# An expert layer whose token rows are turned on VectorE instead of TensorE

## The chip, the cores and the metric

One core of one Trainium2 chip runs the whole program. The metric is the device time of one execution in microseconds (us). Engines are TensorE (matmuls; PE in the profile, its weight loads PEld), VectorE (DVE), ScalarE (ACT), GpSimd (POOL) and SyncE (SP), which issues most DMAs.

## The reference

Three stages in a row on 1536 tokens of 384 features, all fp32: a linear attention, a dense feed-forward layer, and a mixture of eight experts. The change touches the third stage (and the rows that enter it):

```python
def _moe2_ref(x, w_gate, w1, w2, capacity):      # x 1536x384, w1 8x384x1024, w2 8x1024x384
    logits = x @ w_gate
    expert_idx = np.argmax(logits, axis=1)
    ...
    # each expert takes its tokens in order of arrival, up to capacity (384)
    h = np.maximum(np.einsum('ecd,edf->ecf', disp, w1), 0.0)
    y = np.einsum('ecf,efd->ecd', h, w2)
    out[i] = gate_w[i] * y[expert_idx[i], pos[i]]
```

## The kernel before

Each engine has a program of its own, written out by hand, and semaphores tie them together. An engine executes its program in order: what stands behind a wait waits too.

The dense layer ends at about 264 us of the trace. GpSimd has by then scattered each token's row (384 features, its gate, its number) into `slots` in DRAM, by expert. From there the experts 0 to 7 are computed one after the other, 256 slots each (more tokens than that take a branch at the end, which this input doesn't use). Expert e = 2i + r uses the buffers of parity r: the weights of odd experts lie where the dense layer's weights were (`wd_*`), those of even ones in `we_*`. Expert 0 is computed in two tiles of 128 slots by code of its own (`tile_fc1`, `tile_fc2`, `pick_rows`); experts 1 to 7 by `expert(i, r, more)`, where `more` says that another one follows.

Every fp32 product is made of three fp32r matmuls: high by high, high by low, low by high. So each operand is split: ScalarE copies the high part (`_hi`), and VectorE or GpSimd subtracts to get the low part (`_lo`).

Inside an expert, f counts the eight tiles of 128 hidden features:

- TensorE: fc1(f), 9 matmuls of 256 columns into bank f % 2, then from f = 2 on fc2(f - 2), two tiles of slots t, 3 matmuls of 384 columns each, into `ps_ye[t]`. Behind f = F_X = 5 the six transposes `expert_x` of the next expert's rows `xrow` into `ps_xt`. Behind f = 7 come fc2(6) and fc2(7). fc1(f) waits for ge_lo(f - 2), whose bank it overwrites.
- ScalarE: ge_hi(f), the relu of fc1's bank. At f = 2, 3, 4 also a chunk each (1024 columns) of the next expert's W1, at f = 2 after a wait for W1's landing (`s_w1`). At f = 5 the copies of the next x, and from f = 5 on the chunks of W2 (wait `s_w2`).
- VectorE: ge_lo(f); behind it at f = 3, 4, 5 the low part of W1's chunk (L1308), at f = 5 also x_lo (L1293) and the copy of the tokens' numbers to `tok_i` (semaphore tok_ready). After f = 7 `yrow`, the result times the gate (L1321, semaphore ye_ready).
- GpSimd: the low parts of W2's three chunks, then the scatter of the two tiles of `yrow` to `out`.
- SyncE: for each expert the loads of the expert two further on into the buffers of the same parity: W1 (1.5 MB) when all its fc1 are done (he_done), W2 (1.5 MB) when its last fc2 is done (fc2e_done), and the rows x when yrow and tokens have been taken:

```python
                    sp.wait_ge(s_he, ET * (2 * i + r + 1))
                    load_w(2 * i + 2 + r, r)
                    sp.wait_ge(s_fc2e, ET * (2 * i + r + 1))
                    load_w2(2 * i + 2 + r, r)
                    sp.wait_ge(s_ye[r], 2 * (i + 1))
                    sp.wait_ge(s_tok[r], i + 1)
                    load_x(2 * i + 2 + r, r)
```

Of the kernel before, what the change touches and what calls it, by code (L numbers as in the profile page):

```python
# [7 lines left out]
ALU = mybir.AluOpType  # L8
# [4 lines left out]
def build(nc, B, H, S, D, DFF, NE, FE, CAP, rkt_in, nat_in, decay, bonus, bonus_pair, win, wout, wouttr, wgate, wexp, out, slots):  # L13
# [5 lines left out]
    DM = H * D  # L19
# [37 lines left out]
    NOVER = NE + 3  # L57
    LATE = NE * CAP
# [39 lines left out]
    x2t = new("x2t", [128, BT, DM])  # L98
    lg = new("lg", [128, BT, NE])
# [32 lines left out]
    def expert_rows(r):  # L132
        return (new(f"xrow{r}", [128, 2, XR]), new(f"xe_hi{r}", [128, KT, SN], F32R),
                new(f"xe_lo{r}", [128, KT, SN], F32R), new(f"yrow{r}", [128, 2, DM]),
                new(f"tok_i{r}", [128, 2, 1], U32))
# [8 lines left out]
    xrow, xe_hi, xe_lo, yrow, tok_i = zip(rows0, expert_rows(1))  # L144
# [32 lines left out]
    with ctx:  # L177
# [268 lines left out]
        def _(sp):  # L446
# [330 lines left out]
        def _(act):  # L777
# [204 lines left out]
        def _(dve):  # L982
# [273 lines left out]
            def tokens_of(t, s):  # L1256
                dve.wait_ge(s_xr[0], 16 * (t + 1))
                V.tensor_copy(tok_i[0][:, t, :], xrow[0][:, t, TOKEN:XR]).then_inc(s, 1)

            def gated(t, y):  # L1260
                V.tensor_scalar(yrow[0][:, t, :], y, xrow[0][:, t, GATE:GATE + 1], None, ALU.mult).then_inc(s_ye[0], 1)
# [25 lines left out]
            dve.wait_ge(s_y0, 1)  # L1287
            gated(0, ps_y[0][:, 0:DM])

            def expert_x(i, r):  # L1290
                for c, (src, dst) in enumerate(((ps_xt[0][:, :], (0, 2)), (ps_xt[1][:, 0:SN], (2, 3)))):
                    dve.wait_ge(s_xehi[r], 2 * i + c + 1)
                    V.tensor_tensor(xe_lo[r][:, dst[0]:dst[1], :], src.rearrange("p (k n) -> p k n", n=SN),  # L1293
                                    xe_hi[r][:, dst[0]:dst[1], :].bitcast(F32), ALU.subtract).then_inc(s_xelo[r], 1)

            def expert(i, r, more):
                ni, nr = (i, 1) if r == 0 else (i + 1, 0)
                for f in range(ET):
# [17 lines left out]
                for t in range(2):  # L1316
                    if t == 0:
                        dve.wait_ge(s_y0, 2 * i + r + 1)
                    else:
                        dve.wait_ge(s_fc2e, ET * (2 * i + r + 1))  # L1320
                    V.tensor_scalar(yrow[r][:, t, :], ps_ye[t][:, 0:DM], xrow[r][:, t, GATE:GATE + 1], None,  # L1321
                                    ALU.mult).then_inc(s_ye[r], 1)

            tile_row(s_he, ET, s_lrow)
# [10 lines left out]
            dve.wait_ge(s_fc2e, ET)  # L1335
            gated(1, ps_y[0][:, 0:DM])
            expert(0, 1, True)
            with dve.Fori(1, NE // 2 - 1) as i:
                expert(i, 0, True)
                expert(i, 1, True)  # L1340
            expert(NE // 2 - 1, 0, True)
            expert(NE // 2 - 1, 1, False)
# [21 lines left out]
        def _(pe):  # L1364
# [292 lines left out]
            def pick_rows():  # L1657

                pe.wait_ge(s_xr[0], 32)
                for kt in range(KT):  # L1660
                    mm(ps_s[0][:, 128 * kt:128 * kt + 128], xrow[0][:, 1, 128 * kt:128 * kt + 128], ident[:, :],
                       start=kt == 0, stop=False, skip_group_check=True)
                pe.wait_ge(s_pick, 1)
                rows = x2row[(NB - 1) % 2]
                for kt in range(KT):
                    for t in range(BT):
                        last = mm(ps_s[0][:, 128 * kt:128 * kt + 128], rows[:, t, NE + 128 * kt:NE + 128 * kt + 128],
                                  picked[:, t, :], start=False, stop=kt == KT - 1 and t == BT - 1,
                                  skip_group_check=True)
# [14 lines left out]
            def expert_x(i, r):  # L1684
                pe.wait_ge(s_xr[r], 32 * (i + 1))
                if r:
                    pe.wait_ge(s_xelo[0], 2 * (i + 1))
                else:
                    wait_if(pe, s_xelo[1], 2 * i)
                for kt in range(KT):  # L1690
                    for t in range(2):
                        at = (kt % 2) * SN + t * 128
                        last = nc.tensor.transpose(ps_xt[kt // 2][:, at:at + 128],  # L1693
                                                   xrow[r][:, t, 128 * kt:128 * kt + 128], ident[:, :])
                last.then_inc(s_xtr[r], 1)

            def fc2_expert(i, r, f, tiles=(0, 1)):
                pe.wait_ge(s_gelo, ET * (2 * i + r) + f + 1)
                if f == 0:
                    pe.wait_ge(s_ehi[r], 2 * N1 * (i + 1))  # L1700
                    wait_if(pe, s_elo2[r], N1 * (i + r))
                    y_before, n_before = other(s_ye, r, i)
                    wait_if(pe, y_before, 2 * n_before)
                cols = slice(W1 + f * DM, W1 + (f + 1) * DM)
                for t in tiles:
                    g = slice(t * 128, (t + 1) * 128)
# [7 lines left out]
            def expert(i, r, more):  # L1714
                ni, nr = (i, 1) if r == 0 else (i + 1, 0)

                pe.wait_ge(s_elo1[r], N1 * (i + 1) + (0 if r else N1))
                for f in range(ET):
                    q = ET * (2 * i + r) + f
                    wait_if(pe, s_gelo, q if f == 0 else q - 1)  # L1720
# [23 lines left out]
                    if more and f == F_X:  # L1744
                        expert_x(ni, nr)
                if more:
                    fc2_expert(i, r, ET - 2)
                    fc2_expert(i, r, ET - 1)
                else:
# [12 lines left out]
            expert_x(0, 1)  # L1762
# [7 lines left out]
            expert(0, 1, True)  # L1770
            with pe.Fori(1, NE // 2 - 1) as i:
                expert(i, 0, True)
                expert(i, 1, True)
            expert(NE // 2 - 1, 0, True)
            expert(NE // 2 - 1, 1, False)
            pe.wait_ge(s_over, 1)
            over = pe.value_load(n_over[0:1, 0:1], min_val=0, max_val=T)
            with pe.If(over > SN):
                with pe.Fori(0, NOVER) as e:
                    pe.wait_ge(s_dld, 32 * (e + 1))  # L1780
                    for kt in range(KT):
                        last = nc.tensor.transpose(ps_xt[0][:, 128 * kt:128 * kt + 128],
                                                   xrow[0][:, 0, 128 * kt:128 * kt + 128], ident[:, :])
# [93 lines left out]
```

## Time and profile before

| | |
|---|---|
| median of three runs | 415.0 us (414.7 to 415.39) |
| the profiled execution | 415.56 us |
| its span in the trace | 413.7 us |
| TensorE busy | 406.2 us (98%) |
| VectorE, ScalarE, GpSimd busy | 242.4, 188.1, 231.4 us |
| granted TensorE clock | 0.997 of full speed |
| experts 1 to 6 | 285.85 to 391.91 us |

The span is the profiler's, from the first instruction to the last; the execution's own time is longer by what lies around it. Matmuls are pipelined: one of 256 columns is shown as 0.28 us long, but the next starts 0.12 behind it. So the start-to-start distance is what a matmul costs. The same holds to a lesser degree on VectorE and ScalarE, where the next instruction starts up to 0.1 before the end of the last. A wait shows as idle time in brackets with what ended it.

### The profile page before, as it was taken

The page shows a single profiled execution, that of the slowest core. Times are in us where ns is not written, and L with a number is a line of the kernel's source. Part 1 is how long each engine was busy: PE and PEld are TensorE (multiplying, and loading weights), DVE is VectorE, ACT ScalarE, POOL GpSimd, SP SyncE. Part 2 cuts the span into 40 slices and gives each one's busy share as a digit, 9 for nine tenths or more (in the row PEclk, how much of TensorE's full clock was granted, in tenths as well). Part 3 has the DMA queues.
Part 4 walks back from the last instruction along what each step waited for, and adds up shares of the span by engine and source line. Part 5 has one row for each costly group of instructions (what it writes and reads, how often), then busy time and mean ns, then how long its engine had stood idle before and what let it go on. Part 6 is the DMA issues. An engine that isn't in the chain of part 4 may idle for free.

```text
span 413.7 us, 9445 instructions
## 1 busy us (share of the span) xinstructions
PE 406.2 (98%) x3697; PEld 390.3 (94%) x3697; DVE 242.4 (59%) x576; ACT 188.1 (45%) x409; POOL 231.4 (56%) x239
## 2 busy tenths in 40 slices
PE   8999999999999999999999999999999999999995
PEld 8799799999999999999999999999999999999995
DVE  7787955376576547654663487785635546364522
ACT  4786553233333333333343455552645455474420
POOL 3789865567856685668234336065083562826531
PEclk9999999999999999999999999999999999999998
DMA  7998997214030403020018001827383845729000
GB/s 281 399 395 341 348 371 255 72 49 150 10 119 2 139 21 118 2 87 21 2 19 345 2 2 38 326 77 238 135 304 99 346 147 217 279 100 363 8 31 28
DMA packets 18650, 64.98 MB, mean 157 GB/s; under 512 B 2203, under 2 KB 11717, under 8 KB 16432
## 3 DMA queue, kind: packets, MB, share of 16 engines
q1 hardware_dynamic: 16672, 59.67, 39.5%
q0 software_dynamic: 1792, 4.73, 3.0%
q8 instruction: 28, 0.46, 0.5%
q14 instruction: 14, 0.11, 0.1%
q10 hardware_dynamic: 144, 0.00, 0.0%
HBM read 51.98 MB, written 13.21 MB: 158 GB/s over the span
## 4 chain that ended last, share of the span: by engine, by line
PE 88%; DVE 4%; issue 3%; DMA 3%; POOL 1%; ACT 1%; POOLq 0%; SPq 0%; DVEq 0%
PE bank L1369 26%; PE bank L1371 25%; PE bank L1370 24%; PE bank L1390 2%; DMA xrow<-slots 2%; PE bank L1419 1%; PE bank L1455 1%; PE bank L1459 1%; PE bank L1693 1%; PE bank L1448 1%; PE bank L1451 1%; PE bank L1546 1%; PE bank L1728 1%; PE bank L1729 1%; PE bank L1632 1%
## 5 line engine op out<-in xcount | busy, mean ns | idle before, releaser
L707 POOL TENSOR_TENSOR g_lo<-elu,g_hi 128x256 fp32r<-128x256 f32 x95 | 73.7, 777 | 86.9 <-ACT g_hi L882 86.6
L1369 PE MATMUL bank<-xt,wd_hi 128*128 128x256 f32 x285 | 80.5, 283 | 0.6 <-DVE elu L1197 0.6
L1371 PE MATMUL bank<-xt,wd_lo 128*128 128x256 f32 x285 | 80.4, 282 | 0.0
L1370 PE MATMUL bank<-xt,wd_hi 128*128 128x256 f32 x285 | 80.3, 282 | 0.0
L873 ACT ACTIVATE elu<-elu 128x256 f32<-128x256 f32 x96 | 40.1, 418 | 76.4 <-DVE elu L1189 75.9
L1369 PE MATMUL bank<-wd_hi,g_hi 128*128 128x392 f32 (+1 forms) x192 | 67.4, 351 | 0.0
L1371 PE MATMUL bank<-wd_hi,g_lo 128*128 128x392 f32 (+1 forms) x192 | 65.2, 340 | 0.0
L1370 PE MATMUL bank<-wd_lo,g_hi 128*128 128x392 f32 (+1 forms) x192 | 65.1, 339 | 0.0
L1197 DVE SCALAR_TENSOR_TENSOR elu<-elu,bank 128x256 f32<-128x256 f32 x96 | 40.3, 419 | 41.1 <-ACT elu L873 41.1
L882 ACT CAST g_hi<-elu 128x256 fp32r<-128x256 f32 x96 | 39.0, 406 | 44.1 <-DVE elu L1197 44.1
L1369 PEld LDWEIGHTS bank<-xt,wd_hi 128*128 128x128 f32 x285 | 53.9, 189 | 1.2 <-DVE elu L1197 1.1
L1371 PEld LDWEIGHTS bank<-xt,wd_lo 128*128 128x128 f32 x285 | 54.1, 190 | 0.0
L1370 PEld LDWEIGHTS bank<-xt,wd_hi 128*128 128x128 f32 x285 | 54.0, 189 | 0.0
L1301 DVE SCALAR_TENSOR_TENSOR ge_lo<-bank,ge_hi 128x256 fp32r<-128x256 f32 x56 | 23.8, 424 | 48.8 <-ACT ge_hi L940 48.8
L1189 DVE TENSOR_SCALAR elu<-bank 128x256 f32<-128x256 f32 x80 | 33.8, 422 | 31.2 <-PE bank L1371 26.3
L940 ACT ACTIVATE ge_hi<-bank 128x256 fp32r<-128x256 f32 x56 | 21.6, 385 | 53.4 <-PE bank L1371 31.5
L724 POOL TENSOR_TENSOR wd_lo<-wd_raw,wd_hi 128x1024 fp32r<-128x1024 f32 x12 | 30.4, 2559 | 27.5 <-ACT wd_hi L953 24.5
L1369 PEld LDWEIGHTS bank<-wd_hi,g_hi 128*128 128x128 f32 x192 | 36.3, 189 | 2.0 <-POOL g_lo L707 0.8
L724 POOL TENSOR_TENSOR we_lo<-we_raw,we_hi 128x1024 fp32r<-128x1024 f32 x9 | 21.3, 2402 | 27.6 <-ACT we_hi L953 27.6
L1370 PEld LDWEIGHTS bank<-wd_lo,g_hi 128*128 128x128 f32 x192 | 36.4, 190 | 0.0
L1371 PEld LDWEIGHTS bank<-wd_hi,g_lo 128*128 128x128 f32 x192 | 36.0, 188 | 0.0
L729 POOL DMA_INDIRECT out<-yrow,tok_i x16 | 15.7, 982 | 17.4 <-DVE yrow L1321 11.7
(220 smaller groups left out, 943.7 us busy)
## 6 DMA issues: line engine op xcount, KB each, us to landing
we_raw<-wexp SPq DMA_DIRECT2D x8, 1536.0 KB, 6.5
wd_raw<-wexp SPq DMA_DIRECT2D x8, 1536.0 KB, 7.4
rkt<-rkt SPq DMA_DIRECT2D x12, 512.0 KB, 5.7
nat<-nat SPq DMA_DIRECT2D x9, 672.0 KB, 5.4
xrow<-slots SPq DMA_DIRECT2D x16, 193.0 KB, 7.4
wd_raw<-win SPq DMA_DIRECT2D x4, 768.0 KB, 8.6
wd_raw<-wout SPq DMA_DIRECT2D x4, 768.0 KB, 9.0
wo_tr<-wouttr SPq DMA_DIRECT2D x1, 3072.0 KB, 17.6
```

The source lines that it names most:

```text
L707: nc.gpsimd.tensor_tensor(g_lo[:, f % 4, :], elu[:, f % 2, :], g_hi[:, f % 4, :].bitcast(F32), ALU.subtract).then_inc(s_glo, 1)
L724: nc.gpsimd.tensor_tensor(EL[r][:, cols], ER[r][:, cols], EH[r][:, cols].bitcast(F32), ALU.subtract).then_inc(s_elo2[r], 1)
L729: nc.gpsimd.indirect_dma_start(out=out, out_offset=bass.IndirectOffsetOnAxis(ap=tok_i[r][:, t, :], axis=0), in_=yrow[r][:, t, :], in_offse ...
L873: nc.scalar.activation(elu[:, f % 2, :], elu[:, f % 2, :], ACT.Exp, scale=-1.0 if n == 0 else 1.0).then_inc(s_exp, 1)
L882: nc.scalar.copy(g_hi[:, f % 4, :], elu[:, f % 2, :]).then_inc(s_ghi, 1)
L940: nc.scalar.activation(ge_hi[:, f % 4, :], ps_e[f % 2][:, 0:SN], ACT.Relu).then_inc(s_gehi, 1)
L1189: V.tensor_scalar_min(elu[:, f % 2, :], ps_h[f % 2][:, 0:BN], 0.0).then_inc(s_m, 1)
L1197: V.scalar_tensor_tensor(out=elu[:, f % 2, :], in0=elu[:, f % 2, :], scalar=-1.0, in1=ps_h[f % 2][:, 0:BN], op0=ALU.add, op1=ALU.max).then ...
L1301: V.scalar_tensor_tensor(out=ge_lo[:, f % 4, :], in0=ps_e[f % 2][:, 0:SN], scalar=0.0, in1=ge_hi[:, f % 4, :].bitcast(F32), op0=ALU.max, o ...
L1369: mm(dst, w_hi, x_hi, start=start, stop=False)
L1370: mm(dst, w_hi, x_lo, start=False, stop=False)
L1371: return mm(dst, w_lo, x_hi, start=False, stop=stop)
```

## The change

**The rows' load.** `load_x` brought 256 rows in two DMAs of 128 rows. Now the rows come in blocks: four DMAs, each of which brings columns 96p to 96p + 95 of all 256 rows to the 32 partitions from 32p on, row 32b + i to partition 32p + i, block b; and a fifth for gate and token number. In SyncE's loop the load of x stands first, and it waits for the token copy alone.

**The transpose.** TensorE's `expert_x` is gone. VectorE's `expert_cols` turns all 24 squares of 32 by 32 with one instruction, from `xrow` to `xcol` (the storage of `x2t`, free by then), at f = 4. To make 96 columns fill 32 partitions, feature 3q + k becomes row q of the k-th third; the weights W1 are put in the same order by the host (`thirds`), and expert 0's matmul transposes read every third column (`block_cols`).

**The gates.** A copy of the gates to `gate`, beside that of the tokens, so that `xrow` is free earlier.

**The seam.** fc2(6) and fc2(7) of an expert come behind fc1(0) and fc1(1) of the next; VectorE's yrow (`expert_out`) moves behind ge_lo(1) of the next. The first fc2 waits for W2's chunks one by one and for each `ps_ye[t]` by itself.

```diff
+        def block_cols(rows, kt):
+            return rows.rearrange("p (m k) -> p k m", k=KT)[:, kt, :]
+        def xrow_blocks(r):
+            return xrow[r][:, :, :].rearrange("p t c -> p (t c)")[:, 0:2 * DM].rearrange("p (b c) -> p b c", b=8)
...
             def load_x(e, r):
-                for t in range(2):
-                    sp.dma_start(xrow[r][:, t, :],
-                                 slots[bass.ds(e * CAP + t * 128, 128), :]).then_inc(s_xr[r], 16)
+                for p in range(4):
+                    sp.dma_start(xrow_blocks(r)[32 * p:32 * p + 32, :, :],
+                                 slots[bass.ds(e * CAP, SN), 96 * p:96 * p + 96]
+                                 .rearrange("(b i) c -> i b c", i=32)).then_inc(s_xr[r], 16)
+                sp.dma_start(xrow_gt(r), slots[bass.ds(e * CAP, SN), GATE:XR]
+                             .rearrange("(t p) c -> p t c", t=2)).then_inc(s_xr[r], 16)
...
                 for r in range(2):
+                    sp.wait_ge(s_tok[r], i + 1)
+                    load_x(2 * i + 2 + r, r)
                     sp.wait_ge(s_he, ET * (2 * i + r + 1))
                     load_w(2 * i + 2 + r, r)
                     sp.wait_ge(s_fc2e, ET * (2 * i + r + 1))
                     load_w2(2 * i + 2 + r, r)
-                    sp.wait_ge(s_ye[r], 2 * (i + 1))
-                    sp.wait_ge(s_tok[r], i + 1)
-                    load_x(2 * i + 2 + r, r)
...
+            def expert_cols(i, r):
+                dve.wait_ge(s_xr[r], rows_loaded(i, r))
+                V.transpose(xcol.rearrange("p k (b n) -> p b k n", n=32),
+                            xrow_blocks(r).rearrange("p b (n k) -> p b k n", k=KT)).then_inc(s_xtr[r], 1)
...
+                    if f == 1 and behind:
+                        expert_out(bi, br)
...
+                    if more and f == F_X - 1:
+                        expert_cols(ni, nr)
                     if more and f == F_X:
                         expert_x(ni, nr)
                     if f == 5:
-                        dve.wait_ge(s_xr[r], 32 * (i + 1))
+                        dve.wait_ge(s_xr[r], rows_loaded(i, r))
                         wait_if(dve, s_sout[r], 32 * i)
-                        V.tensor_copy(tok_i[r][:, :, :], xrow[r][:, :, TOKEN:XR]).then_inc(s_tok[r], 1)
+                        V.tensor_copy(gate[r][:, :, :], xrow_gt(r)[:, :, 0:1])
+                        V.tensor_copy(tok_i[r][:, :, :], xrow_gt(r)[:, :, 1:2]).then_inc(s_tok[r], 1)
...
+            expert_cols(0, 1)
             tile_row(s_he, ET, s_lrow)
...
                     last.then_inc(s_he, 1)
+                    if f < 2 and behind:
+                        fc2_expert(bi, br, ET - 2 + f)
                     if more and f >= 2:
                         fc2_expert(i, r, f - 2)
...
-                    if more and f == F_X:
-                        expert_x(ni, nr)
-                if more:
-                    fc2_expert(i, r, ET - 2)
-                    fc2_expert(i, r, ET - 1)
```

SyncE's queue, one turn of its loop for the even experts, before (an ISA row computes an address and holds the waits; `wexp` are the weights in DRAM, columns 0 to 3071 W1, the rest W2):

```order
L516 ISA [waits he_done]
L516 DMA we_raw<-wexp 128x3072
L519 ISA [waits fc2e_done]
L519 DMA we_raw<-wexp 128x3072
L552 ISA
L523 ISA [waits tok_ready0,ye_ready0]
L523 DMA xrow_90<-slots 128x386
L523 ISA
L523 DMA xrow_90<-slots 128x386
```

and now:

```order
L537 ISA [waits tok_ready0]
L537 DMA xrow_90<-slots 32x8x96
...
L537 DMA xrow_90<-slots 32x8x96
L540 ISA
L540 DMA xrow_90<-slots 128x2x2
L567 ISA
L530 ISA [waits he_done]
L530 DMA we_raw<-wexp 128x3072
L533 ISA [waits fc2e_done]
L533 DMA we_raw<-wexp 128x3072
```

Five x DMAs and the wait for tok_ready now stand ahead of the wait for he_done and of W1's DMA; they stood behind W2's.

VectorE's queue in the loop, from ge_lo(4) of an even expert to the token copy, before:

```order
L1301 SCALAR_TENSOR_TENSOR ge_lo<-bank,ge_hi 128x256 [waits ge_hi_ready]
L1306 REGISTER_ALU
L1308 TENSOR_TENSOR wd_lo<-wd_raw,wd_hi 128x1024 [waits we_hi_ready1]
L1292 REGISTER_ALU
L1293 TENSOR_TENSOR xe_lo_100<-bank,xe_hi_99 128x512 [waits xe_hi_ready1]
...
L405 REGISTER_ALU [waits xrow_loaded0]
L1315 CAST tok_i_94<-xrow_90 128x2 [waits out_scattered0]
```

and now (the pair of ge_lo and split shown first is that of f = 4):

```order
L1334 SCALAR_TENSOR_TENSOR ge_lo<-bank,ge_hi 128x256 [waits ge_hi_ready]
L1341 REGISTER_ALU
L1343 TENSOR_TENSOR wd_lo<-wd_raw,wd_hi 128x1024 [waits we_hi_ready1]
L1309 ISA
L1310 STREAM_TRANSPOSE x2t<-xrow_99 128x8x3x32 [waits xrow_loaded1]
L1333 REGISTER_ALU
L1334 SCALAR_TENSOR_TENSOR ge_lo<-bank,ge_hi 128x256 [waits ge_hi_ready]
...
L1316 TENSOR_TENSOR xe_lo_101<-x2t,xe_hi_100 128x512 [waits xe_hi_ready1]
...
L1352 COPY gate_95<-xrow_90 128x2 [waits out_scattered0]
L1353 CAST tok_i_94<-xrow_90 128x2
```

The transpose stands ahead of ge_lo(5), the gate copy ahead of the token copy, and x_lo reads the scratchpad instead of a bank.

## Rows read from the trace of the kernel before

**Rows 1.** The page, busy us of each engine, share, instructions.

```profile
PE 406.2 (98%) x3697; PEld 390.3 (94%) x3697; DVE 242.4 (59%) x576; ACT 188.1 (45%) x409; POOL 231.4 (56%) x239
```

**Rows 2.** Timeline of TensorE: start, us, line, operation, out<-in.

```profile
285.85 0.28 PE L1728 MATMUL bank<-xe_hi,wd_hi 128*128 128x256 f32 x1
...
391.91 0.28 PE L1728 MATMUL bank<-xe_hi,wd_hi 128*128 128x256 f32 x1
```

**Rows 3.** Chain that ended last: start, us, what.

```profile
296.67 0.66 PE bank L1693 x6
```

**Rows 4.** TensorE's timeline at a seam, and the chain inside fc2.

```profile
287.83 0.28 PE L1371 MATMUL bank<-xe_hi,wd_lo 128*128 128x256 f32 x1
288.00 0.38 PE L1369 MATMUL bank<-xe_hi,wd_hi 128*128 128x256 f32 x1
...
372.06 0.17 PE bank L1369
```

**Rows 5.** Timeline of TensorE, second tile of expert 0.

```profile
279.95 0.82 PE L1693 MATMUL bank<-ident,xrow 128*128 128x128 f32 x6
280.90 0.66 PE L1632 MATMUL bank<-ident,hrow 128*128 128x128 f32 x4
```

**Rows 6.** Issue to landing, W1 (L516), then W2 (L519), six each.

```profile
DMA to landing us min/median/max: 6.1/6.4/7.7
...
DMA to landing us min/median/max: 6.7/7.9/9.0
```

**Rows 7.** Who waited for whom, 285 to 414: us, times, longest.

```profile
ACT wd_hi L945 <- DMA wd_raw<-wexp: 1.0, 1, 1.0
```

**Rows 8.** Timeline of ScalarE, 298 to 299.

```profile
298.10 1.06 ACT L953 CAST we_hi<-we_raw 128x1024 fp32r<-128x1024 f32 x1
299.06 0.39 ACT L940 ACTIVATE ge_hi<-bank 128x256 fp32r<-128x256 f32 x1
```

**Rows 9.** Timeline of VectorE, 280 to 304, idle before in brackets.

```profile
280.15 0.69 DVE L1249 TENSOR_SCALAR hrow<-bank 128x512 f32<-128x512 f32 x1 [1.23 <-PE bank L1371]
...
283.87 0.14 DVE L1258 CAST tok_i<-xrow 128x1 uint32<-128x1 f32 x1
...
293.97 0.42 DVE L1301 SCALAR_TENSOR_TENSOR ge_lo<-bank,ge_hi 128x256 fp32r<-128x256 f32 x1 [0.54 <-ACT ge_hi L940]
294.31 1.22 DVE L1308 TENSOR_TENSOR we_lo<-we_raw,we_hi 128x1024 fp32r<-128x1024 f32 x1
...
297.98 1.02 DVE L1293 TENSOR_TENSOR xe_lo<-bank,xe_hi 128x512 fp32r<-128x512 f32 x2 [0.35 <-ACT xe_hi L932]
298.91 0.16 DVE L1315 CAST tok_i<-xrow 128x2 uint32<-128x2 f32 x1
...
303.12 1.14 DVE L1321 TENSOR_SCALAR yrow<-bank,xrow 128x384 f32<-128x384 f32 x2 [1.77 <-PE bank L1371]
```

**Rows 10.** VectorE by line: count, busy us, mean ns; splits of W1.

```profile
L1285 DVE TENSOR_TENSOR wd_lo<-wd_raw,wd_hi 128x1024 fp32r<-128x1024 f32 x3 | 5.7, 1955 | 0.0
...
L1308 DVE TENSOR_TENSOR wd_lo<-wd_raw,wd_hi 128x1024 fp32r<-128x1024 f32 x9 | 10.9, 1215 | 0.0
```

**Rows 11.** Timeline of SyncE, 280 to 305, DMA issues.

```profile
280.33 0.35 SPq L516 DMA_DIRECT2D we_raw<-wexp  x1
...
300.65 0.33 SPq L516 DMA_DIRECT2D wd_raw<-wexp  x1
...
304.44 0.86 SPq L523 DMA_DIRECT2D xrow<-slots  x2
```

**Rows 12.** DMA packets between 1.9 and 2.4 us, the startup.

```profile
DMA packets 282, 0.03 MB, mean 69 GB/s; under 512 B 275, under 2 KB 275, under 8 KB 282
```

**Rows 13.** Timeline of GpSimd, the scatter of expert 1's first tile.

```profile
306.52 0.99 POOL L729 DMA_INDIRECT out<-yrow,tok_i  x1 [0.16 <-issue]
```

**Rows 14.** Expert 1's x DMAs: ns, starts, landing.

```profile
L523 SPq DMA_DIRECT2D xrow<-slots x2: 327/381/435, 272.9 to 273.3; - x2
...
DMA to landing us min/median/max: 2.6/2.6/2.7
```

More of the change, by code:

```diff
@@ L143, in build @@
     ge_lo = new("ge_lo", [128, 4, SN], F32R)
-    xrow, xe_hi, xe_lo, yrow, tok_i = zip(rows0, expert_rows(1))
+    xrow, xe_hi, xe_lo, yrow, tok_i, gate = zip(rows0, expert_rows(1))
     wo_tr, end_g = put("wo_tr", [128, KT, DFF], F32, wo_at)
@@ L1287, in _, with expert_out, expert @@
             dve.wait_ge(s_y0, 1)
+            dve.wait_ge(s_atok, 1)
             gated(0, ps_y[0][:, 0:DM])
+            def expert_cols(i, r):
+                dve.wait_ge(s_xr[r], rows_loaded(i, r))
+                V.transpose(xcol.rearrange("p k (b n) -> p b k n", n=32),
+                            xrow_blocks(r).rearrange("p b (n k) -> p b k n", k=KT)).then_inc(s_xtr[r], 1)
             def expert_x(i, r):
-                for c, (src, dst) in enumerate(((ps_xt[0][:, :], (0, 2)), (ps_xt[1][:, 0:SN], (2, 3)))):
+                for c, (lo, hi) in enumerate(((0, 2), (2, 3))):
                     dve.wait_ge(s_xehi[r], 2 * i + c + 1)
-                    V.tensor_tensor(xe_lo[r][:, dst[0]:dst[1], :], src.rearrange("p (k n) -> p k n", n=SN),
-                                    xe_hi[r][:, dst[0]:dst[1], :].bitcast(F32), ALU.subtract).then_inc(s_xelo[r], 1)
-            def expert(i, r, more):
+                    V.tensor_tensor(xe_lo[r][:, lo:hi, :], xcol[:, lo:hi, :],
+                                    xe_hi[r][:, lo:hi, :].bitcast(F32), ALU.subtract).then_inc(s_xelo[r], 1)
+            def expert_out(i, r):
+                dve.wait_ge(s_tok[r], i + 1)
+                for t in range(2):
+                    if t == 0:
+                        dve.wait_ge(s_y0, 2 * i + r + 1)
+                    else:
+                        dve.wait_ge(s_fc2e, ET * (2 * i + r + 1))
+                    V.tensor_scalar(yrow[r][:, t, :], ps_ye[t][:, 0:DM], gate[r][:, t, :], None, ALU.mult).then_inc(s_ye[r], 1)
+            def expert(i, r, more, behind):
                 ni, nr = (i, 1) if r == 0 else (i + 1, 0)
+                bi, br = (i - 1, 1) if r == 0 else (i, 0)
                 for f in range(ET):
@@ L1312, in expert @@
                     if f == 5:
-                        dve.wait_ge(s_xr[r], 32 * (i + 1))
+                        dve.wait_ge(s_xr[r], rows_loaded(i, r))
                         wait_if(dve, s_sout[r], 32 * i)
-                        V.tensor_copy(tok_i[r][:, :, :], xrow[r][:, :, TOKEN:XR]).then_inc(s_tok[r], 1)
[L1316 to L1322, printed above, removed]
+                        V.tensor_copy(gate[r][:, :, :], xrow_gt(r)[:, :, 0:1])
+                        V.tensor_copy(tok_i[r][:, :, :], xrow_gt(r)[:, :, 1:2]).then_inc(s_tok[r], 1)
+                if not more:
+                    expert_out(i, r)
+            expert_cols(0, 1)
             tile_row(s_he, ET, s_lrow)
@@ L1682, in _, with w2_chunk @@
             last.then_inc(s_y0, 1)
[L1684 to L1695, printed above, removed]
+            def w2_chunk(f):
+                return -(-(f + 1) * DM // ECH)
             def fc2_expert(i, r, f, tiles=(0, 1)):
                 pe.wait_ge(s_gelo, ET * (2 * i + r) + f + 1)
[L1699 to L1703, printed above, removed]
+                if w2_chunk(f) > w2_chunk(f - 1):
+                    pe.wait_ge(s_ehi[r], 2 * N1 * (i + 1) - N1 + w2_chunk(f))
+                    wait_if(pe, s_elo2[r], N1 * (i + r) - N1 + w2_chunk(f))
                 cols = slice(W1 + f * DM, W1 + (f + 1) * DM)
                 for t in tiles:
+                    if f == 0:
+                        y_before, n_before = other(s_ye, r, i)
+                        pe.wait_ge(y_before, 2 * n_before - 1 + t)
                     g = slice(t * 128, (t + 1) * 128)
@@ L1712, in fc2_expert, with expert @@
                     last.then_inc(s_fc2e, 1)
-            def expert(i, r, more):
+            def expert(i, r, more, behind):
                 ni, nr = (i, 1) if r == 0 else (i + 1, 0)
+                bi, br = (i - 1, 1) if r == 0 else (i, 0)
                 pe.wait_ge(s_elo1[r], N1 * (i + 1) + (0 if r else N1))
@@ L1743, in expert @@
                                 fc2_expert(i, r, f - 2 - t, (t,))
-                    if more and f == F_X:
-                        expert_x(ni, nr)
-                if more:
-                    fc2_expert(i, r, ET - 2)
-                    fc2_expert(i, r, ET - 1)
-                else:
+                if not more:
                     for t in range(2):
@@ L1850 @@
     w_in = moe_w_in[order].reshape(DM // 128, 128, DFF // 128, 128).transpose(1, 2, 0, 3).reshape(128, -1)
+    thirds = [DM // 128 * p + kt for kt in range(DM // 128) for p in range(128)]
     gate_pad = np.zeros((DM, 32), np.float32)
```

49 lines of the change are left out of this document (28 added, 21 removed).

## Prediction

> **What bounds the kernel now.** I read the page first: TensorE is busy 98% of the span and no other engine above 59% [rows 1], so the kernel is a row of matmuls and every other engine matters only through what it makes TensorE wait for. Then TensorE's timeline over the seven experts: the first fc1 matmul of expert 1 starts at 285.85 and that of expert 7 at 391.91 [rows 2]. That is 106.06 us for six periods, 17.68 each. The chain of waits shows what the change can take out of a period: six transposes of expert rows, 0.66 [rows 3]. At the seam next to nothing is lost: from the last matmul of fc1(1) to the first of fc1(2) is 0.17 in all, of which I count 0.05 as idle [rows 4]. So if all else kept up, six periods would lose 6 x 0.71 = 4.3 us. The first transposes, at 279.95, win nothing: they lie inside TensorE's wait for hrow, which lasts to 280.90 either way [rows 5].
>
> **The part that moves.** The stream of weights has next to no slack. ScalarE waits for W1 of the next expert at f=2, in line ahead of ge_hi(3). Before, W1 is issued 0.3 behind the last fc1 and lands 6.1 to 7.7 later, median 6.4 [rows 6]; once already ScalarE sat 1.0 on it [rows 7]. Now SyncE's queue holds, ahead of that W1, a wait for tok_ready of the current expert and five DMAs. tok_ready comes from VectorE at f=5, behind everything that hangs on the W1 just landed: the split of the chunks, the transpose, x_lo, two copies. So a ring closes: W1 lands, ScalarE, VectorE, token copy, SyncE, five x DMAs, next W1. Its length, not TensorE's, is the period when it is longer than TensorE's 17.0 (17.68 less 0.71).
>
> **The ring's length, step by step.** From W1's landing: ScalarE splits chunk 0, and ge_hi(3) starts 0.96 behind it (298.10 to 299.06) and takes 0.38 [rows 8]; with 0.05 to wake and 0.04 to VectorE, ge_lo(3) starts at +1.43. VectorE then never rests. ge_lo to the next instruction is 0.34 (293.97 to 294.31); a split is 1.22 busy [rows 9, 10] and, with the same 0.08 of overlap, 1.14 start to start; x_lo is 0.93 (297.98 to 298.91) [rows 9]. Three ge_lo 1.02, three splits 3.42, x_lo 0.93, gate copy and token copy 0.25.
>
> The transpose has no row. 768 columns at a split's rate (1024 in 1215 ns) [rows 10] are 0.91 in proportion, an estimated 0.95 busy with a fixed part, 0.87 start to start: the low end, since an instruction that reads and writes each column once has nothing to gain on the split. The high end is 1.8, twice that, if 4-byte data in strided blocks go at half rate; the splits that ran beside GpSimd, 1955 ns instead of 1215 [rows 10], are the only row of such a slowing. I take 0.87, as the row with most alike (fp32, scratchpad to scratchpad, one stream out). Sum from landing to token copy: 1.43 + 1.02 + 3.42 + 0.93 + 0.25 + 0.87 = 7.9. Then 0.2 to the first x DMA, as from yrow's end at 304.26 to 304.44 [rows 9, 11].
>
> X, the delay of W1 by the five x DMAs. Two of the old ones stand 0.53 apart (0.86 for both, each 0.33) [rows 11], so five cost 2.65 in issue alone: the low end. They hold 1280 pieces (4 x 256 of 384 B, 256 of 8 B) where the old two held 256. In the startup 282 packets of two queues, 275 of them under 512 B, came in 0.5 us [rows 12]: 1.8 ns a packet, or about 3.6 for one queue. At that rate 1280 pieces keep the queue 4.6 us, and W1 stands behind them: the high end. I take 3.4, nearer to the issue pace, since a startup of two queues at once is a poor row for a rate.
>
> W, issue to landing of W1: 6.1 to 7.7 [rows 6]. I take 6.8, above the median, because W1, issued 3 to 4 later than before, now flies while GpSimd scatters two tiles of out; before they began at 306.52, 5.9 behind W1's issue at 300.65 [rows 13, 11]. W2's landings, which share the queue with such traffic, range from 6.7 to 9.0 [rows 6].
>
> The Trainium skill (DMA: Bandwidth & Descriptors, Specifications) wants at least 512 B for line rate and says that below this a read-modify-write is done; its section on the anatomy of one DMA calls descriptor generation small, with many descriptors before the cost shows. By the second alone X would be the 2.65 of issue and the sum +0.1, no change; by the first X moves to its high end. No row here shows a load of this kind.
>
> **The sum.** Write Z = X + W = 10.2. The first token copy of the ring, for expert 0, ends at 283.87 + 0.14 [rows 9], 284.35 with the gate copy (0.15) and the wake (0.2). This one is worse than later ones: W1 of expert 2 was issued right behind the last fc1 of expert 0, at 280.33 [rows 11]. Now it lands at 284.35 + 10.2 = 294.55. Each later W1 lands 8.1 + 10.2 = 18.3 behind the one ahead; the sixth, for expert 7, at 386.05. Expert 7 starts when ge_lo(6) of expert 6 is done, which stands right behind the token copy: 7.9 + 0.4 later, 394.35. At that point 12 fc2 matmuls are still owed that before lay ahead of the seam, 12 x 0.17 = 2.1 [rows 4]. So 394.35 + 2.1 - 391.91 = +4.5. In general it is 6Z - 56.7: no change at Z = 9.4; TensorE's own pace, and no further gain, from about Z = 8.7; with a slower transpose add 6 x the excess. The tail behind expert 7's start has no transposes and keeps its length.
>
> **Costed at nothing.** The deferred fc2(6) and fc2(7) are as many matmuls as before. expert_out moves behind ge_lo(1); its two yrow, 1.14 together [rows 9], fit before fc2(0) wants the banks, by about 0.3, since TensorE has 2.1 of work in between; if late, each lateness is TensorE's. The x loads themselves land long before f=4 of the next expert. The softer waits on W2's chunks win nothing where no W2 wait is seen, and W2, behind W1 in the queue, is wanted only after x_hi. The early transposes of expert 0's rows now read their stationary side every third column: 21 matmuls of 0.11 (six take 0.66) [rows 3], doubled, are +2.3 at the worst; at equal cost 0. I take 0, since the loads of the weights overlap the matmuls. expert_cols(0, 1) stands ahead of hrow on VectorE, which was free 1.23 there, up to hrow's start at 280.15 [rows 9]; the x rows, issued from 272.9 and landing in 2.6 [rows 14], now X later, are there at 278.9, and the transpose ends at 279.85, 0.3 before hrow's start; at the high end of X it is a microsecond late.
>
> **Time.** The profiled execution took 415.56 for a span of 413.7; the median of the runs is 415.0, and I add to that: **419.5 us**.
>
> **Rivals.** (a) *Faster.* Z stays under 9.4: five issues cost 2.65 and W1 lands in 6.1 to 6.6. Then Z = 8.75 to 9.25, the change -4.3 to -1.2: 410.7 to 413.8. For it: the median of 6.4 and the issue pace [rows 6, 11]. Against: it needs pieces of 384 B to cost nothing and no scatter in W1's way. 0.26. (b) *No change*, Z within 0.15 of 9.4: 0.06. (c) *The forecast*, Z from 9.6 to 11.5, 416 to 427: 0.54. (d) *Worse*: the transpose at 1.8 gives +5.6 more, 425; both X and W at their high ends, 4.6 + 7.7 = 12.3, give +17, 432. 0.14. The low and high ends together are 410.7 and 432, and 437 with the slow transpose. (e) That the transposes don't leave TensorE can't be: the order shows them gone.
>
> A gain or loss under 0.2% (0.8 us) is what a measurement can't tell from no change. **Range** 411 to 428: about 1 in 10 lies under it, inside (a), and 1 in 10 above, inside (d). The forecast case alone is 416 to 427. Slower 0.68, same 0.06, faster 0.26.
>
> **What would show it.** Right: ScalarE waits of 3 to 5 us for W1 by DMA at L945 and its twin in each expert but the last; W1 issued 3 or more behind the last fc1; TensorE idle about 1 in each period, at fc1(5) or at the next expert's start on ge_lo, and first fc1s 18.3 apart. Each term is a row: transpose 0.95, five issues, W1's landing. Wrong: first fc1s 17.0 apart and no ScalarE wait (a), or a transpose row near 1.8 (d). What would make it wrong otherwise is a stall of hrow over 1 us, or expert_out blocking fc2(0).

## The result, and the profile after

The changed kernel takes 431.19 us (median of 5 runs, 430.24 to 431.94) against 415.22 (5 runs beside it): 1.0384 times the time before [1.0373, 1.0396]. The forecast was 419.5, range 411 to 428. The direction came true, the size did not: the loss is 16.0 us, not 4.5. Of the six executions of the experiment w_x_w2_gate_f4 below, two (425.62, which is the profiled one, and 428.04) lie over 1.5% above its fastest and are left out of its time and ratio.

The page of the changed kernel, against [rows 1]: TensorE is as busy as before in microseconds and idle for the rest; VectorE is 18 us busier, far more than seven transposes and seven copies should cost.

```profile
PE 407.0 (95%) x3655; PEld 389.6 (91%) x3655; DVE 260.7 (61%) x592; ACT 187.0 (44%) x409; POOL 232.9 (54%) x239
```

TensorE's timeline after, first fc1 matmul of experts 1, 2, 4 and 7 (before: [rows 2]):

```profile
286.80 0.28 PE L1755 MATMUL bank<-xe_hi,wd_hi 128*128 128x256 f32 x1
...
306.69 0.57 PE L1755 MATMUL bank<-xe_hi,we_hi 128*128 128x256 f32 x1 [2.25 <-DVE ge_lo L1334]
...
345.73 0.38 PE L1755 MATMUL bank<-xe_hi,we_hi 128*128 128x256 f32 x1 [2.26 <-DVE ge_lo L1334]
...
404.66 0.35 PE L1755 MATMUL bank<-xe_hi,wd_hi 128*128 128x256 f32 x1 [1.55 <-issue]
```

The six periods are 117.86 in all, 11.80 more than the 106.06 before. The 2.07 of fc2 work that the new order puts behind each seam is still owed at that point, and expert 1 starts 0.95 later: 11.80 + 2.07 + 0.95 = 14.8, which is the growth of the span (413.7 to 428.5).

The waits of the changed kernel, 270 to 430 us (engine, line, releaser: us in all, times, longest), against [rows 7]: ScalarE now waits for W1 for each of the six experts, as predicted, for 1.5 to 5.3.

```profile
ACT we_hi L961 <- DMA we_raw<-wexp: 11.0, 3, 5.3
...
ACT wd_hi L961 <- DMA wd_raw<-wexp: 6.4, 3, 2.8
PE bank L1755 <- DVE ge_lo L1334: 7.7, 4, 2.3
```

One turn of the ring can be read off four timelines. ScalarE, the start and the end of the turn (W1 has just landed in both):

```profile
335.07 1.05 ACT L961 CAST we_hi<-we_raw 128x1024 fp32r<-128x1024 f32 x1 [2.89 <-DMA we_raw<-wexp]
...
354.50 1.05 ACT L961 CAST wd_hi<-wd_raw 128x1024 fp32r<-128x1024 f32 x1 [2.84 <-DMA wd_raw<-wexp]
```

VectorE between them:

```profile
336.43 0.42 DVE L1334 SCALAR_TENSOR_TENSOR ge_lo<-bank,ge_hi 128x256 fp32r<-128x256 f32 x1 [3.80 <-ACT ge_hi L956]
...
339.37 1.21 DVE L1310 STREAM_TRANSPOSE x2t<-xrow 128x768 f32<-128x768 f32 x1
340.50 0.38 DVE L1334 SCALAR_TENSOR_TENSOR ge_lo<-bank,ge_hi 128x256 fp32r<-128x256 f32 x1
340.80 1.21 DVE L1343 TENSOR_TENSOR we_lo<-we_raw,we_hi 128x1024 fp32r<-128x1024 f32 x1
341.93 1.02 DVE L1316 TENSOR_TENSOR xe_lo<-x2t,xe_hi 128x512 fp32r<-128x512 f32 x2
342.87 2.33 DVE L1352 COPY gate<-xrow 128x2 f32<-128x2 f32 x1
345.12 0.16 DVE L1353 CAST tok_i<-xrow 128x2 uint32<-128x2 f32 x1
```

GpSimd (the first of its three splits of W2) and SyncE at the same place:

```profile
342.58 2.59 POOL L740 TENSOR_TENSOR we_lo<-we_raw,we_hi 128x1024 fp32r<-128x1024 f32 x1 [8.45 <-ACT we_hi L969]
```

```profile
345.47 1.84 SPq L537 DMA_DIRECT2D xrow<-slots  x4
347.49 0.40 SPq L540 DMA_DIRECT2D xrow<-slots  x1
348.14 0.35 SPq L530 DMA_DIRECT2D wd_raw<-wexp  x1
```

The turn is 10.40 from the landing to the first x DMA, 2.67 to W1's issue and 6.36 to the landing: 19.43, where 8.1, 3.4 and 6.8 were predicted. The row that nobody expected is the gate copy: two columns, 2.33 us. It starts 0.29 behind GpSimd's first split of W2 and ends at 345.20, 0.03 behind the end of that split at 345.17. In six of seven experts it is so; in the last, beside which no split runs, it takes 0.16 (count, then ns least/median/most):

```profile
L1352 DVE COPY gate<-xrow x7: 158/2331/2360, 303.8 to 416.7; 128x2 f32<-128x2 f32 x7
```

### The profile page after: what moved, and what is told of

It reads as the page before. It is cut to its first block, busy times and chain, and to the rows that moved or that the text cites. A ratio compares the mean times of both kernels' runs of the same rounds, so it can differ in the third digit from the quotient of the medians.

```text
span 428.5 us, 9450 instructions
## 1 busy us (share of the span) xinstructions
PE 407.0 (95%) x3655; PEld 389.6 (91%) x3655; DVE 260.7 (61%) x592; ACT 187.0 (44%) x409; POOL 232.9 (54%) x239
## 4 chain that ended last, share of the span: by engine, by line
PE 74%; DVE 11%; issue 6%; DMA 5%; ACT 1%; SPq 1%; POOL 1%; DVEq 0%; POOLq 0%; ACTq 0%
PE bank L1404 21%; PE bank L1406 20%; PE bank L1405 20%; DMA we_raw<-wexp 3%; PE bank L1425 2%; DMA wd_raw<-wexp 2%; DVE we_lo L1343 1%; DVE gate L1352 1%; PE bank L1454 1%; DVE wd_lo L1343 1%; DVE xe_lo L1316 1%; PE bank L1490 1%; PE bank L1494 1%; DVE ge_lo L1334 1%; DVE x2t L1310 1%
## 5 line engine op out<-in xcount | busy, mean ns | idle before, releaser
L1334 DVE SCALAR_TENSOR_TENSOR ge_lo<-bank,ge_hi 128x256 fp32r<-128x256 f32 x56 | 22.8, 415 | 58.8 <-ACT ge_hi L956 58.8
```

## The experiments

Time and ratio of each are against the kernel before, run on the same chip.

**gate_f4** moves the gate copy from f = 5 to f = 4, right behind the transpose.

```diff
+                    if f == F_X - 1:
+                        dve.wait_ge(s_xr[r], rows_loaded(i, r))
+                        V.tensor_copy(gate[r][:, :, :], xrow_gt(r)[:, :, 0:1])
                     if more and f == F_X:
...
-                        V.tensor_copy(gate[r][:, :, :], xrow_gt(r)[:, :, 0:1])
```

> The changed kernel with one edit: the gate copy stands at f = 4 behind the transpose, before GpSimd begins its splits, instead of at f = 5. Theory A (a closed ring from W1's landing over the token copy to the next W1 sets the period, and the gate copy, held up 2.2 us while GpSimd splits W2, is a link of it): the copy takes 0.15, six periods of 19.4 to 19.9 shrink by 2.2 each to about 17.2, the time falls by 13, from 431.2 to about 418. Theory B (the ring is set by the five x DMAs and W1's landing, and the gate copy only fills time that would be waited anyway): the copy is short and the time stays within 1 us of 431.

Measured: 434.56 us, 1.0464 [1.0418, 1.051], slower still; both theories missed. The copy itself is 0.12 at its new place, but the block moved on to its neighbours. VectorE:

```profile
340.15 0.12 DVE L1349 COPY gate<-xrow 128x2 f32<-128x2 f32 x1
...
341.65 3.22 DVE L1316 TENSOR_TENSOR xe_lo<-x2t,xe_hi 128x512 fp32r<-128x512 f32 x2
344.80 2.30 DVE L1355 CAST tok_i<-xrow 128x2 uint32<-128x2 f32 x1
```

The token copy, now the first copy there, takes 2.30 to 2.36 in all six turns. In two of them, the one shown and the fifth, x_lo is blocked as well: its two pieces take 3.22 instead of 1.02, and the token copy behind it stands through the next split. From one landing of W1 to the next it is 19.5 to 19.9, and 21.6 and 22.0 in those two turns. So x_lo and a cast pay too; it isn't the gate copy's own doing.

**gate_cast** makes the gate tile fp32r, so that the copy is a cast; the two readers of the tile take it back as fp32. The gates are rounded by it.

```diff
-new(f"gate{r}", [128, 2, 1]))
+new(f"gate{r}", [128, 2, 1], F32R))
```

> The changed kernel with the gate copy left at f = 5 but written as fp32r (so the gates are rounded to that type): the instruction becomes a CAST like the token copy behind it, with the same source, size and place. If what is held up by GpSimd is this kind of instruction (a plain fp32 COPY from scratchpad to scratchpad), the row takes 0.15 and the time is about 418, as with the copy at f = 4. If any instruction of VectorE at that place waits for GpSimd's split (or for the source), it still takes 2.3 and the time stays at 431.

Measured: 432.09 us, 1.0392 [1.0366, 1.0419], as the changed kernel. The cast is blocked like the copy:

```profile
342.69 2.35 DVE L1352 CAST gate<-xrow 128x2 fp32r<-128x2 f32 x1
344.95 0.16 DVE L1353 CAST tok_i<-xrow 128x2 uint32<-128x2 f32 x1
```

**w_x_w2** opens the ring: SyncE issues W1 first, then waits for tok_ready.

```diff
-                    sp.wait_ge(s_tok[r], i + 1)
-                    load_x(2 * i + 2 + r, r)
                     sp.wait_ge(s_he, ET * (2 * i + r + 1))
                     load_w(2 * i + 2 + r, r)
+                    sp.wait_ge(s_tok[r], i + 1)
+                    load_x(2 * i + 2 + r, r)
```

> The changed kernel with one edit in SyncE's loop: wait he_done and W1's DMA first, then the wait for tok_ready and the five x DMAs, then W2; the gate copy stays at f = 5. Theory A: the ring is cut, W1 is issued 0.35 behind the last fc1 again and ScalarE waits under 0.5 for it. The gate copy, started about 1.3 before GpSimd's first chunk ends, then costs about 0.1 to 0.3 a period. Periods about 17.1, time 412 to 413. Theory B (small pieces slow the weights behind them in the queue, wherever they stand): W2 lands late instead, ScalarE waits for W2 at f = 5, time 416 or more.

Measured: 418.45 us, 1.0072 [1.0056, 1.0089]. ScalarE's waits for W1 are gone and with them 12.7 us, as theory A has it. Its time of 412 to 413 was missed: the gate copy is still 2.35, here at 354.14, and delays ge_lo(6), for which TensorE waits 0.9 to 1.0 in each of the six periods where 0.1 to 0.3 was expected. So the ring and the block are two things. Outside the ring the block makes a period 18.0 instead of the 16.8 of early (below), 1.2 more; inside it costs 2.3 (pool_waits). TensorE:

```profile
356.94 0.39 PE L1755 MATMUL bank<-xe_hi,wd_hi 128*128 128x256 f32 x1 [0.90 <-DVE ge_lo L1334]
```

**w_x_w2_gate_f4** is both edits.

> Both edits: SyncE issues W1, x, W2, and the gate copy stands at f = 4. Theory A: TensorE sets the period, 17.0 (17.68 less six transposes of 0.66 and the seam), so 6 x 0.7 = 4.2 under the kernel before, plus 1.0 which the strided weight loads of expert 0's rows cost: 411.5 to 412.3. Theory B: as without the gate edit, 416 or more.

Measured: 418.6 us in the median of four, 1.0083 [1.0066, 1.01]. Theory A was missed, as in gate_f4: in the one trace the token copy takes 2.30 to 2.36 in all six turns, and x_lo 3.25 in two. Theory B had the time but not the cause: no wait of ScalarE for a weight shows.

**pool_waits** leaves VectorE and SyncE as changed, and makes GpSimd wait with its W2 splits until the current expert's token copy is done.

```diff
             with pool.Fori(1, NE // 2 - 1) as i:
+                pool.wait_ge(s_tok[0], i + 1)
                 split_w2(i, 1)
                 scatter_out(i, 0)
+                pool.wait_ge(s_tok[1], i + 1)
                 split_w2(i + 1, 0)
```

(and likewise for the first and the last)

> The changed kernel with one edit, on GpSimd alone: it waits for tok_ready of the current expert before it begins the splits of W2. The two runs before moved the gate copy and changed its kind, and the 2.3 us moved to x_lo and to the token copy behind it. Theory A: a VectorE instruction that reads the scratchpad by both ports can't start while a split on GpSimd runs and waits for that one instruction's end (up to 2.4 us). With GpSimd held back, gate copy and token copy take 0.15 each and x_lo 1.0, each ring is 2.2 shorter, 17.2 instead of 19.4, and the time is 431.2 - 13 = about 418, though GpSimd starts later. Theory B: it is the read of xrow itself (a small strided piece that DMA wrote) or a short instruction behind x_lo that takes 2.3: the rows stay at 2.3 and the time at 431.

Measured: 417.40 us, 1.0051 [1.0035, 1.0066]: 13.8 us back from the changed kernel, 6 x 2.3. VectorE, then GpSimd right behind it:

```profile
373.52 0.16 DVE L1356 COPY gate<-xrow 128x2 f32<-128x2 f32 x1
373.58 0.16 DVE L1357 CAST tok_i<-xrow 128x2 uint32<-128x2 f32 x1
```

```profile
373.92 7.11 POOL L740 TENSOR_TENSOR we_lo<-we_raw,we_hi 128x1024 fp32r<-128x1024 f32 x3 [8.02 <-DVE tok_i L1357]
```

No instruction of VectorE, ScalarE or SyncE was changed; only GpSimd's splits start later, behind the token copy instead of 0.29 ahead of the gate copy. That shows the cause of the excess: a 128x2 copy of VectorE that starts behind one of GpSimd's splits isn't done until that split ends.

**early** keeps the change's SyncE order and moves VectorE's and ScalarE's x work ahead of GpSimd's splits: transpose at f = 2, gate copy, token copy and x_hi at f = 3, x_lo at f = 4. VectorE's part of the edit (ScalarE's `expert_x` moves from F_X to F_X - 2):

```diff
-                    if more and f == F_X - 1:
+                    if more and f == F_X - 3:
                         expert_cols(ni, nr)
-                    if more and f == F_X:
+                    if more and f == F_X - 1:
                         expert_x(ni, nr)
-                    if f == 5:
+                    if f == F_X - 2:
                         dve.wait_ge(s_xr[r], rows_loaded(i, r))
```

> The changed kernel with VectorE's and ScalarE's pieces drawn forward inside an expert, SyncE's order as in the change: transpose at f = 2, gate and token copies and x_hi at f = 3, x_lo at f = 4, all before GpSimd's splits begin. Theory A: no VectorE row is held up, tok_ready comes 3 us behind W1's landing, so the ring is 3.1 + 0.2 + 2.7 + 6.4 = 12.4 and binds nobody; TensorE sets the period at 17.0. Time 415.1 - 6 x 0.7 + 1.0 (strided weight loads for expert 0) = 411.5 to 412.3. Theory B (small pieces slow W1, or the transpose or the deferred work holds TensorE up somewhere else): ScalarE still waits for W1, 415 or more.

Measured: 415.56 us, 1.0002 [0.9993, 1.0011], no difference from before. First fc1s are 16.80 apart in five of the six periods (323.07, 339.87, ... 390.27), but 19.07 in the first: W1 of expert 2 still stands behind expert 0's token copy and five x DMAs, and ScalarE waits 5.4 for it. The expectation of 411.5 to 412.3 had left that one turn out; without the wait that period is 14.86 (early_w_first).

**early_natural** also reads expert 0's rows in contiguous columns, with a copy of expert 0's weights laid out for it (entry NE + 1 of `wexp`); the other experts are untouched.

```diff
-block_cols(xrow[0][:, 0, 0:DM], kt), ident[:, :])
+xrow[0][:, 0, 128 * kt:128 * kt + 128], ident[:, :])
...
-            load_w(0, 0)
+            load_w(NE + 1, 0)
```

> As the kernel with the pieces drawn forward, and expert 0 reads its rows in the natural order of features (contiguous stationary operand), with a copy of its weights in that order from the host. If the 0.95 us by which expert 1 starts later in the changed kernel (286.80 against 285.85) are the 21 transposes and picks with every third column as stationary operand, they go back to 0.11 each and the time is 0.9 to 1.1 under the kernel without this edit, 410.5 to 411.3. If the delay has another source (the transpose ahead of hrow), nothing changes.

Measured: 414.57 us, 0.9981 [0.9972, 0.999]: 1.0 less than early, as expected. TensorE grouped by line and shape, 262 to 290 us (count | busy us, mean ns), the changed kernel:

```profile
L1702 PE MATMUL bank<-picked,x2row 128*128 128x128 f32 x12 | 2.3, 338 | 0.0
...
L1696 PE MATMUL bank<-ident,xrow 128*128 128x128 f32 x6 | 1.2, 328 | 0.0
```

and early_natural:

```profile
L1702 PE MATMUL bank<-picked,x2row 128*128 128x128 f32 x12 | 1.5, 275 | 0.0
...
L1696 PE MATMUL bank<-ident,xrow 128*128 128x128 f32 x6 | 0.8, 274 | 0.0
```

**turn_plain** is early_natural with a transpose that reads 32 neighbouring columns. It leaves out the order by thirds: the features of experts 1 to 7 then stand in another order than the weights', so the output is another.

```diff
-rearrange("p b (n k) -> p b k n", k=KT)).then_inc(s_xtr[r], 1)
+rearrange("p b (k n) -> p b k n", k=KT)).then_inc(s_xtr[r], 1)
```

> As the one before, but VectorE's transpose reads 32 neighbouring columns per square instead of every third, so that the experts' features are in the wrong order. If the strided read is why 768 columns take 1.22 us (768 at a split's rate would be 0.95), the row falls to about 0.95. If the squares of 32 by 32 cost it, the row stays at 1.2.

Measured, one run: 414.49 us. The transposes of the two kernels, early_natural first (ns, least/median/most):

```profile
L1310 DVE STREAM_TRANSPOSE x2t<-xrow x7: 1216/1218/1247, 279.1 to 378.4; 128x768 f32<-128x768 f32 x7
```

```profile
L1310 DVE STREAM_TRANSPOSE x2t<-xrow x7: 962/967/969, 279.1 to 378.3; 128x768 f32<-128x768 f32 x7
```

Read contiguously it is about the 0.95 of the prediction; every third column costs 0.25 more. Off the ring, as here, that is worth nothing that one run shows (414.57 with the stride).

**early_w_first** is early_natural with SyncE's first turn taken out of the loop: for expert 2 alone W1 goes ahead of the token wait and the x DMAs (`True` in `loads`).

```diff
+            loads(0, 0, True)
+            loads(0, 1)
+            with sp.Fori(1, NE // 2 - 1) as i:
+                loads(i, 0)
+                loads(i, 1)
```

> The kernel with the pieces drawn forward and expert 0 in natural order, and SyncE's first turn taken out of the loop: for expert 2 it issues W1 ahead of the x rows, since expert 0's token copy comes late (285) and its last fc1 early (280). In the kernel without this edit ScalarE waits 5.2 us for that W1 and TensorE stands 2.4 + 1.2 in the first period, 18.82 instead of 16.8 + what is deferred. Theory A: those 3.6 us go, six periods of 16.8, expert 7 starts near 385.4: 414.6 - 3.6 = 411.0, 1.0% under the kernel before. Rival: the x rows of expert 2, now behind its W1 in the queue, land too late for the transpose at f = 2 of expert 1, and VectorE's wait gives back 1 us or more: 412 or above.

Measured: 410.44 us (409.88 to 410.66) beside 415.76, 0.987 [0.9853, 0.9886]: faster than both kernels, by 1.3% and 4.8%. SyncE's first turn, and the page:

```profile
280.38 0.35 SPq L530 DMA_DIRECT2D we_raw<-wexp  x1
284.35 1.90 SPq L537 DMA_DIRECT2D xrow<-slots  x4
```

```profile
PE 400.2 (98%) x3655; PEld 385.1 (94%) x3655; DVE 249.5 (61%) x592; ACT 188.5 (46%) x409; POOL 234.4 (57%) x239
```

TensorE is back at 98%, and the span is 4.1 less than early_natural's (408.7 and 412.8), where 3.6 was expected. The five full periods are 16.80 each. Before they were 17.68 in the mean, 17.6 to 17.7 but for the last, 17.93, in which ScalarE waits 1.0 for W1. So taking the transposes off TensorE and changing the seam, which no run here tells apart, is worth 0.8 to 0.9 a period once nothing else is late.

**x_in_ten** loads the same x rows in ten DMAs instead of five, in pieces of the same size and number.

```diff
-                for p in range(4):
+                for half in range(2):
+                    for p in range(4):
+                        b = slice(4 * half, 4 * half + 4)
```

> The changed kernel with the same x rows in ten DMAs instead of five (each half of the slots by itself), the same 1024 pieces of 384 B and 256 of 8 B. Theory A: what the x rows add to the ring is the time to issue them, 0.54 each, and not their pieces: W1 is issued 5.3 to 5.5 behind the token copy instead of 2.7, still lands 6.4 later, each ring is 2.7 longer, 22.1, and the time 431.2 + 6 x 2.7 = 447. Rival: the pieces set it (1280 at 3.6 ns), the issues lie inside that time, and the time stays within 3 us of 431.

Measured: 450.96 us, 1.0854 [1.0836, 1.0872], 19.8 more than the changed kernel. SyncE:

```profile
333.52 1.84 SPq L539 DMA_DIRECT2D xrow<-slots  x4
335.54 0.35 SPq L542 DMA_DIRECT2D xrow<-slots  x1
336.09 1.82 SPq L539 DMA_DIRECT2D xrow<-slots  x4
338.09 0.35 SPq L542 DMA_DIRECT2D xrow<-slots  x1
338.72 0.35 SPq L530 DMA_DIRECT2D we_raw<-wexp  x1
339.26 0.33 SPq L533 DMA_DIRECT2D we_raw<-wexp  x1
```

From the first x DMA to W1's issue it is 5.20, 2.53 more, and 6 x 2.53 = 15.2 (expected 6 x 2.7). The ring passes on each DMA issued in it; the count of issues is X, not the pieces. The other 4.6 go with W1's landing, which was expected to stay: ScalarE starts on it 7.5 behind its issue in the mean of six, against 6.8 in the changed kernel (6 x 0.8 = 4.7). The traces show what goes with it. In five of these turns W2's DMA is issued 0.5 behind W1's, as shown, and in four of the five W1 takes 7.8 to 8.5 (6.8 in the other). In the changed kernel that is so in the first turn alone, with 8.1; where W2 comes 2.1 or more behind, W1 takes 6.2 to 7.1. No experiment moved W2 by itself, so this isn't shown to be the cause.

## Why the prediction was wrong

**The mechanism was right.** The period is the closed ring from W1's landing through the token copy and the x DMAs to the next W1's: ScalarE waits for each of the six W1s, opening the ring takes its waits away (w_x_w2), and lengthening it lengthens the kernel (x_in_ten).

**The step that failed** is in the sum of the ring's length: "gate copy and token copy 0.25". The two, with the wake to the first x DMA, take 2.60 (342.87 to 345.47) where 0.25 and 0.2 were put, 2.15 too little in each turn. pool_waits takes just that away, and the kernel gets 13.8 us faster: without the block it comes out at 417.4, inside the forecast case. Before, the token copy at 298.91 [rows 9] was just ahead of GpSimd's first split of that expert, at 299.25. GpSimd's timeline of before:

```profile
299.25 7.12 POOL L724 TENSOR_TENSOR we_lo<-we_raw,we_hi 128x1024 fp32r<-128x1024 f32 x3 [11.34 <-ACT we_hi L953]
```

The split waits for ScalarE's first W2 chunk, which stands behind x_hi. ScalarE's x_hi, before and after:

```profile
297.36 0.59 ACT L932 CAST xe_hi<-bank 128x512 fp32r<-128x512 f32 x1 [1.32 <-PE bank L1693]
```

```profile
340.61 0.62 ACT L948 CAST xe_hi<-x2t 128x512 fp32r<-128x512 f32 x1 [1.78 <-DVE x2t L1310]
```

GpSimd's split starts 1.90 behind x_hi's start before and 1.97 behind it after. But before, VectorE had ge_lo(5) and its third W1 split behind it and waited for x_hi; now it makes the transpose first, which releases x_hi, and owes both. So the first copy comes 2.26 behind x_hi's start instead of 1.56. A margin of 0.34, the same in all six turns before, became -0.29. The prediction priced the copies from a row that had won that race, and never asked when GpSimd starts.

**The sign had been there.** [rows 10] has three splits with a mean of 1955 ns, which I read as a slowing beside GpSimd. They aren't alike; VectorE and GpSimd of the kernel before:

```profile
274.97 3.43 DVE L1285 TENSOR_TENSOR wd_lo<-wd_raw,wd_hi 128x1024 fp32r<-128x1024 f32 x1
```

```profile
273.92 3.40 POOL L724 TENSOR_TENSOR wd_lo<-wd_raw,wd_hi 128x1024 fp32r<-128x1024 f32 x1 [2.95 <-ACT wd_hi L914]
```

GpSimd's split ends at 277.32; VectorE's, begun 1.05 behind it, ends at 278.40, 1.08 later, about the 1.14 that a split takes start to start. The other two took 1.22 each, as anywhere. That is one instruction that stood still, not three slow ones. GpSimd's own split was held likewise, 3.40 instead of 2.4, since VectorE's split ahead of it ran to 275.05. By that reading a two-column copy that starts behind a split costs what is left of it, up to 2.4 us, and six of them 13. The Trainium skill (SBUF — State Buffer, Who interferes with whom) says that VectorE and GpSimd share a pair of ports under an exclusive lock, and that the one who issues second blocks for the whole instruction. It names copies and casts, and VectorE instructions with two inputs in the scratchpad when GpSimd's reads the scratchpad too. The rows agree: copy 2.33, cast 2.35 and 2.30, x_lo 3.22 blocked; ge_lo, at most 0.69, and yrow, at most 0.62, which read a bank, never.

**The other terms.** The transpose is 1.13 start to start, not 0.87, for its stride of 12 bytes (turn_plain): +1.6 over six turns. X is 2.67, not 3.4: pure issue, the pieces of 384 B cost nothing that shows. So of the prediction's two readings of the Trainium skill (DMA: Bandwidth & Descriptors) the one that gave 2.65 has the number, and the cost below 512 B doesn't show here; but the section behind that one, the anatomy of one DMA, describes DMAs issued from GpSimd, and these are SyncE's. W is 6.4 in the median, not 6.8, scatters or no. Together (0.26 - 0.73 - 0.44) these give back 0.9 a turn. The ring is 19.43 = 18.3 + 2.15 + 0.26 - 0.73 - 0.44, less 0.1 of small terms. The first W1 of the ring came 1.4 late (296.00 against 294.55): the token copy was 0.9 late and its DMA took 8.1, the longest, less 0.7 of X. The last came at 394.00, five turns of 19.60 in the mean, and expert 7 starts 10.66 behind it instead of 8.3, the block once more. Together 1.45 + 6.50 + 2.36 = 10.3, which is what expert 7's start, 404.66, is behind the predicted 394.35.

**Costed at nothing.** The stationary operand read every third column isn't free: 338 ns against 275 in 12 matmuls and 328 against 274 in six, and expert 1 starts 0.95 later; early_natural takes 1.0 away. The stated bound of +2.3 held it. The gain was put at 0.71 a period and is 0.8 to 0.9. expert_out and the deferred fc2 cost nothing that shows: in early_w_first every full period is 16.80.

**The rivals.** (a) lived on Z under 9.4, and Z was 9.0: it would still have been about level, since the +0.95 and the slower transpose take its gain; pool_waits says +0.5%. (d) named two causes, neither of which came; the loss of its size came from a third.

## What to carry to other kernels

Before a small copy is put into a chain that others wait on, look at what GpSimd is doing at that microsecond: beside a split the copy's price was what was left of the split, not its own 0.1 us. A mean over a group that is far above its twin's is to be opened into single rows first, for a block and a slowing give the same mean and opposite forecasts. And a load that must be early is issued ahead of any wait for work that hangs on the load before it; here the order that wins is the one where the transposes and copies stand before GpSimd's splits and the first W1 before the first token wait.

## What the runs showed of the hardware

- A block may hit one instruction or two in a row. In the changed kernel the token copy behind the blocked gate copy slips in at once (0.16) though two more splits follow; its row starts at 345.12, the next split's at 345.14. In gate_f4 the next split starts at 344.54, ahead of the token copy at 344.80, and the copy stands through it (2.30). So in these rows the one that starts first goes first, and GpSimd pays as well: its split takes 2.59 instead of 2.38 where x_lo's second piece still ran (342.54 to 342.95), and 3.13 in early, begun at 369.83 beside VectorE's W1 split of 369.48 to 370.69.
- VectorE's transpose isn't blocked. The first one of the changed kernel lies inside a GpSimd split and takes 1.24, as against 1.21 to 1.22 of the others. VectorE, then GpSimd:

```profile
279.82 1.24 DVE L1310 STREAM_TRANSPOSE x2t<-xrow 128x768 f32<-128x768 f32 x1
```

```profile
278.25 3.38 POOL L740 TENSOR_TENSOR wd_lo<-wd_raw,wd_hi 128x1024 fp32r<-128x1024 f32 x1
```

- A fp32 transpose of 128x768 on VectorE takes 0.97 contiguous and 1.22 at a stride of three columns; a 128x128 fp32 stationary operand at that stride makes its matmul 0.06 longer. The Trainium skill (SBUF — State Buffer, Door 1) calls strides of up to four fp32 free; these rows differ, and they decide.
- TensorE's granted clock fell behind two of TensorE's six stalls at a first fc1. Stretches of the changed kernel around the wait that ends at 306.69 (us, busy and count of TensorE, its weight loads, VectorE, ScalarE, GpSimd, then granted clock, DMA share, GB/s):

```profile
304.00:306.00 2.00, 0.44 (x3) 0.12 (x1) 2.00 (x1) 1.87 (x3) 2.00 (x1) 1.00 0.00 0
306.00:307.50 1.50, 0.81 (x4) 0.82 (x5) 0.88 (x4) 0.00 (x0) 1.50 (x2) 0.69 0.04 7
307.50:309.00 1.50, 1.50 (x8) 1.50 (x8) 0.00 (x0) 0.00 (x0) 1.50 (x2) 0.50 0.88 187
309.00:312.00 3.00, 3.00 (x19) 3.00 (x19) 0.42 (x1) 0.75 (x2) 1.79 (x1) 0.83 0.86 211
```

After 2.25 idle it stood at half, 1.2 GHz, in the stretch from 307.5 to 309 and was back at full from 312 on. After a stall just as long (2.26, up to 345.73) it stayed at 1.00. Over the whole execution the mean is 0.989 against 0.997 before.
